# Attention and two MoE layers in one program: three w_out products moved from step 4 to step 5, and with them a wait and an order on two other engines

## What is computed

```
attention:  scores = q k^T / 8 over 2 batches x 8 heads x 768 positions x 64; keep the window of 128
            positions and the 4 first keys ("sinks"); softmax; times v
layer 1:    h = x w_in (512 -> 1024); solu = h * softmax(h); ln = (solu - mean)/std * g; x2 = ln w_out (1024 -> 512)
layer 2:    h = x2 w2_in (512 -> 2048); out = relu(h)^2 w2_out (2048 -> 512)
```

## Time and profile before

| | us |
|---|---|
| median of 3 runs (lowest to highest) | 483.87 (483.83 to 484.03) |
| profiled execution | 483.68 |
| its span in the trace | 481.7 |
| TensorE busy in it | 472.0 (98%) |
| VectorE busy | 280.4 (58%) |
| ScalarE busy | 213.1 (44%) |
| GpSimd busy | 102.6 (21%) |

### The profile page before, as it was taken

One profiled execution on the slowest core, in us unless ns is written; L12 is line 12 of the kernel. 1 busy time (PEld: TensorE's weight loads), 2 busy tenths in 40 slices (PEclk: granted clock), 3 DMA queues, 4 the chain that ended last, 5 costly groups with the idle time before them and its releaser, 6 DMA issues.

```text
span 481.7 us, 7313 instructions
## 1 busy us (share of the span) xinstructions
PE 472.0 (98%) x2636; PEld 383.0 (80%) x2636; DVE 280.4 (58%) x490; ACT 213.1 (44%) x562; POOL 102.6 (21%) x153
## 2 busy tenths in 40 slices
PE   7999999999999999999999999999999999999997
PEld 6667787877788888878888888888888888888885
DVE  4999889899989888767755354322222233222232
ACT  4787876665777666242324253222222232222222
POOL 2365423320321232739930000000000000000000
PEclk9999999999999999999999999999999999999999
DMA  8921437766478424497300000200000020000002
GB/s 213 324 88 46 144 100 197 229 167 191 112 199 202 111 57 120 119 258 234 90 0 0 1 1 1 87 0 0 0 0 0 0 87 1 0 0 1 0 1 87
DMA packets 51670, 41.80 MB, mean 87 GB/s; under 512 B 28024, under 2 KB 37496, under 8 KB 51128
## 3 DMA queue, kind: packets, MB, share of 16 engines
q1 hardware_dynamic: 51032, 40.74, 29.8%
q10 hardware_dynamic: 608, 0.66, 0.5%
HBM read 30.38 MB, written 11.01 MB: 86 GB/s over the span
## 4 chain that ended last, share of the span: by engine, by line
PE 92%; DVE 3%; POOL 2%; DMA 1%; ACT 1%; issue 0%; ACTq 0%; DVEq 0%; POOLq 0%
PE score_ps L1619 27%; PE h_ps L1633 14%; PE w_ps L1460 13%; PE h_ps L1420 12%; PE w_ps L1633 7%; PE wt_ps L1633 7%; PE o_ps L1386 4%; PE score_ps L1352 2%; PE wt_ps L1352 2%; PE h_ps L1437 1%; PE wt_ps L1363 1%; DMA x2T<-qT 1%; PE o_ps L1407 1%; POOL pT_own L552 1%; POOL pT_earlier L556 1%; DVE prob L1061 1%
## 5 line engine op out<-in xcount | busy, mean ns | idle before, releaser
L1619 PE MATMUL score_ps<-x2T_hi,w2in_hi 128*128 (+1 forms) x192 | 74.8, 389 | 0.0
L1619 PE MATMUL score_ps<-x2T_hi,w2in_lo 128*128 (+1 forms) x192 | 74.7, 389 | 0.0
L1619 PE MATMUL score_ps<-x2T_lo,w2in_hi 128*128 (+1 forms) x192 | 74.7, 389 | 0.0
L1279 DVE TENSOR_TENSOR e<-e 128x512 f32<-128x512 f32 x24 | 17.9, 744 | 82.0 <-ACT e L937 82.0
L1279 DVE TENSOR_TENSOR sq<-relu 128x512 f32<-128x512 f32 x24 | 17.2, 718 | 76.9 <-ACT relu L937 76.8
L937 ACT ACTIVATE relu<-score_ps 128x512 f32<-128x512 f32 x24 | 14.3, 597 | 90.4 <-PE score_ps L1619 90.4
L937 ACT ACTIVATE e<-score_ps 128x512 f32<-128x512 f32 x24 | 14.4, 599 | 89.7 <-PE score_ps L1619 89.7
L1619 PEld LDWEIGHTS score_ps<-x2T_lo,w2in_hi 128*128 128x128 f32 x192 | 36.1, 188 | 7.5
L1619 PEld LDWEIGHTS score_ps<-x2T_hi,w2in_lo 128*128 128x128 f32 x192 | 36.0, 188 | 7.4
L1619 PEld LDWEIGHTS score_ps<-x2T_hi,w2in_hi 128*128 128x128 f32 x192 | 36.0, 187 | 7.4
L712 ACT ACTIVATE prob<-sm,nbias 128x132 f32<-128x132 f32 (+1 forms) x96 | 37.7, 394 | 0.8
(11 more groups left out here) (189 smaller groups left out, 1096.5 us busy)
## 6 DMA issues: line engine op xcount, KB each, us to landing
u_dram<-uT SPq DMA_DIRECT2D x18, 256.0 KB, 3.3
lnT_raw<-u_dram SPq DMA_DIRECT2D x36, 128.0 KB, 2.8
w2in<-w_in SPq DMA_DIRECT2D x4, 1024.0 KB, 5.3
w2out<-w_out SPq DMA_DIRECT2D x8, 512.0 KB, 10.2
V<-v SPq DMA_DIRECT2D x12, 256.0 KB, 3.3
x2T<-x_dram SPq DMA_DIRECT2D x12, 256.0 KB, 4.7
x_dram<-x SPq DMA_DIRECT2D x44, 64.0 KB, 2.2
k_raw<-kT SPq DMA_DIRECT2D x20, 132.0 KB, 2.8
```

Source lines behind the costliest of these rows:

```text
L1279: nc.vector.tensor_tensor(sq[f % 2], relu[f % 2], relu[f % 2], ALU.mult).then_inc(sq_ready, 1)
L1619: done = mm(h2_ps[f % 2], ws[:, c, fs], xs[:, c, bass.ts(blk, BLK)], start=(c == 0 and i == 0), stop=(c == MC - 1 and i == 2))
```

## The change

It has four parts. On TensorE, step 4 makes only product 20 at its end, and the products 21 to 23 of tile 3 (the last of the eight chunks of w_out, three products) stand in step 5 behind the second scores of tile 7. In `score`, the wait for the copies of p moves from head pair 0 to head pair 1. On ACT, in step 5 alone, the copies of the scores of pairs 2 and 3 stand ahead of all three roundings of ln, and the first rounding is moved behind the rounding of x. On DVE, in step 2 alone, `normalize_p(4, 1)` stands ahead of the second maximum of h instead of behind `nhmax`.

```diff
--- before.py
+++ after.py
@@ -787,18 +787,23 @@
 
 
                 n = t + 1
-                if t > EARLY:
+                if t > EARLY and not alone(n):
                     round_lnT(t - 1, 0)
                 copy_earlier(t + 2, 0)
                 copy_earlier(t + 2, 1)
                 if t + 3 < NT:
                     round_q(t + 3)
                 round_xT(n)
+                if alone(n):
+                    copy_earlier(t + 2, 2)
+                    copy_earlier(t + 2, 3)
+                    round_lnT(t - 1, 0)
                 if t > EARLY:
                     round_lnT(t - 1, 1)
                     round_lnT(t - 1, 2)
-                copy_earlier(t + 2, 2)
-                copy_earlier(t + 2, 3)
+                if not alone(n):
+                    copy_earlier(t + 2, 2)
+                    copy_earlier(t + 2, 3)
                 if normalized_by_act(t):
                     normalize_hidden(t)
                 bias(t + 2, 0)
@@ -1134,9 +1139,12 @@
                     split_q(t + 3)
                 normalize_p(t + 2, 0)
                 hidden_max(n, 0)
+                if t == EARLY:
+                    normalize_p(t + 2, 1)
                 hidden_max(n, 1)
                 hidden_max_all(n)
-                normalize_p(t + 2, 1)
+                if t > EARLY:
+                    normalize_p(t + 2, 1)
                 if t + 3 < NT:
                     split_k(t + 3)
                 gate_and_norm(n)
@@ -1329,7 +1337,7 @@
                     pe.wait_ge(k_split, n)
                 if merges(n) and p == 0:
                     pe.wait_ge(merged, merges(n))
-                if p == 0 and n >= EARLY + 2:
+                if p == 1 and n >= EARLY + 2:
                     pe.wait_ge(pT_copied, GROUPS * n)
                 if p == 0 and sink_tiles(n):
                     pe.wait_ge(p_sinkT_copied, sink_tiles(n))
@@ -1500,6 +1508,8 @@
                 ahead = 0 if alone(n) else 3
                 if ahead:
                     project(t - 1, first, first + ahead)
+                else:
+                    project(t - 2, 21, 24)
                 pe.wait_ge(u_ready, 2 * t + 2)
                 hidden(n, 0, 24)
                 project(t - 1, first + ahead, 18)
@@ -1508,7 +1518,7 @@
                 project(t - 1, 18, 20)
                 if has_sinks(t + 2):
                     transpose_sinks(t + 2)
-                project(t - 1, 20, 24)
+                project(t - 1, 20, 21 if alone(n + 1) else 24)
 
             def last_step():
```

## The result

| | before | changed |
|---|---|---|
| median of 9 runs, us | 484.13 | 486.98 |
| lowest to highest | 483.83 to 485.92 | 485.12 to 489.07 |
| ratio (95% interval) | | 1.0052 (1.0036 to 1.0068) |
| profiled execution, us | 483.68 | 488.05 |
| its span, us | 481.7 | 486.1 |

The change makes the kernel slower, by 2.5 us on the ratio (1.7 to 3.3). Forecast were 485.2 and a range up to 485.9: the sign was right, the size was not, and the median lies outside the range.

The account below looks back on a forecast made before the run. TensorE, holding 92% of the chain of waits, was taken as the bound. +1.15 and +0.23 gave +1.38 on the profiled 483.68, or 485.06; that execution lay 0.19 under the median, so 485.2, range 483.6 to 485.9.

Parts of the forecast that it names:

- Step 2, the late chain on ScalarE (+1.15): End of step 2: second maximum queued behind the normalization makes ScalarE's exponential of h and TensorE's sink values late, +1.15 us.
- The early transposes: Step 2: second transposes of p start 0.69 us earlier, but TensorE then stands 1.9 us, so nothing is gained.
- Steps 4 and 5 (+0.23): Held products delay VectorE's x2 transpose, and the delay reaches the last normalization of p that TensorE awaits: +0.23 us.
- The wait a head pair later and ScalarE's order: Wait for copies of p moved by a pair costs nothing in other steps; ScalarE's step 5 swap keeps the same instructions.
- The clock behind the stand: TensorE's 1.9 us stand in step 2 might drop its clock to 1.2 GHz; left out of the sum, chance 0.03.
- The rival: Clock falls after the step 2 stand: 9 to 16 products at 0.21 more each, +1.9 to +3.4, 487.1 to 488.6; chance 0.03.
- the two upper bounds: Step 2 at most +1.22 us; steps 4 and 5 at most +0.58 if the second scores come no earlier.

Follow-up runs that it names:

- experiment with work in VectorE's hole: The change without its VectorE part of step 2, plus normalization of h of tile 5 put ahead of VectorE's x2 transpose in step 5; 484.11 us, ratio 0.9999.
- experiment with the rest of the change: The change without its VectorE part: held products, wait a head pair later, ScalarE's order of step 5, on the kernel before; 484.09 us, ratio 1.0007.
- e6_sum_behind_copies: Held products, moved wait, step 5 normalization of h ahead of x2 transpose, plus ScalarE's sum behind the copies in steps 2 to 9; 484.41 us, ratio 0.9997.

## Why the prediction was wrong

*Step 2, the late chain on ScalarE (+1.15): right.* 1.11 and 1.13 in the two profiles of the changed kernel, and 1.12 or 1.13 in the four experiments that have this order. The early transposes bought nothing.

*Steps 4 and 5 (+0.23): right in mechanism, 0.06 too large.* 0.17 to 0.18, passed on through VectorE. The second scores came 0.40 earlier instead of 0.35, hence the held products ended earlier than I put them. The experiment with work in VectorE's hole showed VectorE's list to be the carrier. In step 6, 0.14 was given back (16.29 against 16.43), for which the sum had no term. ScalarE's wait for the load of ln there went from 1.2 to 0.7, so what came later came off a wait; that this is the reason is not shown by a run of its own.

*The wait a head pair later and ScalarE's order: right at nothing*, as far as the experiment with the rest of the change can tell: its steps 2 and 3, which have the moved wait, take 14.90 and 16.33 against 14.88 and 16.33. ScalarE's order in step 5 was in no run without the held products, so its share of the 0.17 isn't known.

*The clock behind the stand: wrong.* This is the step that failed. The prediction worked out that TensorE would stand 1.9 us, twice its longest stand before, and then left the clock out of the sum and gave it a chance of 0.03, because no row showed such a stand. The clock fell in 12 of 18 executions and cost 1.61 us in the trace. The rival had put 1.9 to 3.4 on it, from a guess of 9 to 16 products at the slower pace for which no row gave a reason; the measured cost lies under its lower end. With 1.15 + 0.23 + 1.61 = 2.99 over 483.87 the time would have been 486.9; the median is 486.98. That this agrees so well is partly luck, since the kernel before came out at 484.13 in the same runs and the measured lengths add up to 2.7. The prediction named the rule of the Trainium skill (TensorE: Matmul & The Clock Gate, Part 1) that the throttled clock is the default and activity releases it. The trace agrees with that: 0.50 from about 81.8 to 85.2. An absent row was read as evidence against a fall, when the change itself made the first case in which it could come. The term should have stood in the range, and with a chance that the absence of a row does not make small.

*The range* left out the clock on purpose, and with it the result. Its upper end of 485.9 is also not the sum of the two upper bounds, which is 485.67 (483.87 + 1.22 + 0.58). And it allowed for no scatter upwards: single runs of the kernel before took up to 2.1 us more than its median, and the profiled executions differ by up to 1.64 us in the start-up alone.

## What to carry to other kernels

Before an instruction is moved forward in an engine's list, ask what that instruction itself waits for, and what it then holds up: here the second normalization waited for ScalarE and held up the maximum that ScalarE was waiting for. When a change lengthens a stand of TensorE, count the stand and the half clock that can follow it as two terms, even if the trace has no example of the second. And a gain won in one step has to be followed into the next: of the 0.57 us won in steps 4 and 5, 0.43 was lost again in step 6 until the order of SyncE's stores was changed too.

## What the runs showed of the hardware

After a stand of 1.89 us between stretches of work, the granted clock was 0.50 for 3.4 us (81.8 to 85.2 in one profile). In it one group of eight values followed the other after 0.86 us (82.44 to 83.30), against 0.44 at full clock (79.36 to 79.80 in the kernel before). By the mean clock it fell in 12 of 18 executions of the changed kernel. The fall came 1.3 to 1.6 us after TensorE was back at work, in three profiles, and not in the stand. With a stand of 1.20 us (by the profiled execution) it fell in 2 of 12 executions, with 0.3 us in 0 of 11 in one kernel and 1 of 9 in another. Where no long stand was added it fell too, rarely: in 1 of 12 of e6_sum_behind_copies, and in 1 of the 81 runs of the kernel before in the three sets. Where in the program those single falls were isn't known. Seven useless products of 512 columns in the stand took 1.61 us off the step behind it; in the two kernels with them the clock fell in 1 of 20 executions. The profile's granted clock reads 1.00 for the first products of the program, although they follow each other at half the later pace, 0.44 against 0.23 us; in the later fall the granted clock and the pace agree.
